# Gather ids loaded one tile ahead, and row transposes moved amid the second layer of the tile in front

## The reference, cut to what matters

```python
logits = x @ w_gate + modality_bias[modality_id]
e_idx = np.argmax(logits, axis=1)          # one expert per token
gate_w = probs[np.arange(N), e_idx]
for e in range(E):
    mask = e_idx == e
    h = np.maximum(x[mask] @ w1[e], 0.0)   # 512 -> 1024
    out[mask] = gate_w[mask, None] * (h @ w2[e])   # 1024 -> 512
```

## Time and profile before

| | |
|---|---|
| device time, 3 runs | 541.74, 542.89, 543.88 us (median 542.89) |
| profiled execution, its own time | 546.48 us |
| span of its trace | 544.8 us |
| PE busy | 519.8 us, 95% of the span |
| DVE, ACT, POOL busy | 215.7, 205.0, 220.1 us |
| mean granted clock of PE | 0.984 |

### The profile page before, as it was taken

How to read it: one execution, slowest core, us unless ns; L and a number is a source line. 1 busy time by engine, 2 the same in 40 slices (tenths; PEclk the granted TensorE clock), 3 DMA queues, 4 the chain that set the end, 5 groups by cost and what they waited for, 6 DMA issues and landing times. The chain is left out here.

```text
span 544.8 us, 9123 instructions
## 1 busy us (share of the span) xinstructions
PE 519.8 (95%) x2966; PEld 427.9 (79%) x2967; DVE 215.7 (40%) x418; ACT 205.0 (38%) x353; POOL 220.1 (40%) x222
## 2 busy tenths in 40 slices
PE   3999999999999999999999999999989999999993
PEld 2878888888788888878888888778768888888872
DVE  3433333333436322223623666362212472222892
ACT  0143333333343444444344655222212452222880
POOL 3675555454333365533347552130120161112461
PEclk9699999999999999999999999999989999999998
DMA  6944433430020700008100003105871111111110
GB/s 204 410 179 155 156 134 137 154 83 5 1 78 1 278 30 1 0 11 320 55 0 2 0 1 109 28 25 196 285 247 40 39 31 48 39 39 39 39 37 2
DMA packets 23017, 49.54 MB, mean 91 GB/s; under 512 B 8775, under 2 KB 10447, under 8 KB 22992
## 3 DMA queue, kind: packets, MB, share of 16 engines
q1 hardware_dynamic: 16496, 41.83, 21.7%
q0 software_dynamic: 2896, 7.36, 4.3%
q10 hardware_dynamic: 3600, 0.03, 0.3%
HBM read 42.80 MB, written 7.20 MB: 92 GB/s over the span
## 5 line engine op out<-in xcount | busy, mean ns | idle before, releaser
L520 POOL TENSOR_TENSOR wi_lo<-wd_raw,wi_hi 128x512 fp32r<-128x512 f32 x48 | 62.0, 1292 | 144.1 <-ACT wi_hi L660 144.0
L1245 PE MATMUL psum<-xT,wi_lo 128*128 128x512 f32 x192 | 77.3, 402 | 0.0
L1253 PE MATMUL psum<-wo_hi,act_lo 128*128 128x512 f32 x192 | 75.7, 394 | 0.4 <-DVE act_lo L911 0.4
L1247 PE MATMUL psum<-xT,wi_hi 128*128 128x512 f32 x192 | 75.0, 391 | 0.0
L1246 PE MATMUL psum<-xT,wi_hi 128*128 128x512 f32 x192 | 74.8, 390 | 0.0
L1255 PE MATMUL psum<-wo_hi,act_hi 128*128 128x512 f32 x192 | 74.8, 390 | 0.0
L1254 PE MATMUL psum<-wo_lo,act_hi 128*128 128x512 f32 x192 | 74.7, 389 | 0.0
L908 DVE SCALAR_TENSOR_TENSOR act_f<-psum,act_f 128x512 f32<-128x512 f32 x48 | 33.1, 690 | 95.4 <-ACT act_f L678 94.9
L678 ACT ACTIVATE act_f<-psum 128x512 f32<-128x512 f32 x48 | 28.6, 597 | 97.3 <-PE psum L1247 97.3
L525 POOL TENSOR_TENSOR wo_lo<-wd_raw,wo_hi 128x512 fp32r<-128x512 f32 x48 | 61.9, 1289 | 2.7 <-ACT wo_hi L665 2.7
L1334 PE MATMUL psum<-we_hi,he_lo 128*128 128x512 f32 x120 | 48.9, 408 | 4.2 <-issue 3.7
(11 more groups left out here) (167 smaller groups left out, 825.3 us busy)
## 6 DMA issues: line engine op xcount, KB each, us to landing
we_raw<-w_exp SPq DMA_DIRECT2D x32, 512.0 KB, 5.3
wd_raw<-w_dense SPq DMA_DIRECT2D x16, 512.0 KB, 5.4
qk_in<-attn_qk SPq DMA_DIRECT2D x10, 512.0 KB, 3.3
kv_in<-attn_kv SPq DMA_DIRECT2D x10, 512.0 KB, 4.2
x_d<-x_sb SPq DMA_DIRECT2D x12, 256.0 KB, 2.2
qk_more<-attn_qk SPq DMA_DIRECT2D x2, 512.0 KB, 6.4
kv_more<-attn_kv SPq DMA_DIRECT2D x2, 512.0 KB, 7.0
decay_mask<-pow_d SPq DMA_DIRECT2D x2, 256.0 KB, 3.7
```

What stands on the lines that cost most here:

```text
L520: nc.gpsimd.tensor_tensor(wi_lo[:, r, :], dense_raw(f, 0), wi_hi[:, r, :].bitcast(F32), ALU.subtract).then_inc(s_wil, 1)
L1245: nc.tensor.matmul(h, w_lo, hi, start=(c == 0), stop=False)
L1247: mm = nc.tensor.matmul(h, w_hi, hi, start=False, stop=(c == DC - 1))
L1253: nc.tensor.matmul(bank(ACC + i), lo, wo_hi[:, r, :], start=first, stop=False)
```

## The change

Ids. A second ids buffer, ids_n, receives the load from slots_d. POOL copies it to ids_g (a copy of 128x2) once the ids have landed and the gather before has landed, and gathers from ids_g. A new semaphore, s_idc, counts these copies. ACT's load of the ids of tile t+3 now waits for the copy for tile t+2 (before: the load for t+2 waited for the landing of gather t+1), and stands behind rows(t+1) on ACT. The table has one more entry (NTAB is 24, was 23), and one more load is made.

Transposes. In body, down(t, 0) is cut in two halves of 6 matmuls and transposes(t+1) stands between them; transposes(t+2) at the end is gone. So rows on ACT and rows_lo on DVE move from the end of iteration t (for tile t+2) into iteration t (for tile t+1): in a switch iteration they stand behind the first four weight pieces, in another at the iteration's start. For tiles 1 and 2 the same is written out. No rows beyond the last tile are transposed any more.

```diff
-NTAB = MAX_TILES + PRE + 1
+NTAB = MAX_TILES + PRE + 2
...
             def gather(t):
+                pool.wait_ge(s_ids, 16 * t)
+                pool.sem_inc(s_pass, 1)
+                pool.wait_ge(s_gat, 16 * t)
+                pool.sem_inc(s_pass, 1)
+                nc.gpsimd.tensor_copy(ids_g[:], ids_n[:]).then_inc(s_idc, 1)
+                pool.wait_ge(s_idc, t + 1)
+                pool.sem_inc(s_pass, 1)
                 pool.wait_ge(s_et, t)
-                pool.sem_inc(s_pass, 1)
-                pool.wait_ge(s_ids, 16 * t)
                 pool.sem_inc(s_pass, 1)
                 pool.indirect_dma_start(out=xg[:], ...
...
 ACT, ahead of the loop:
-            load_ids(ids_g, PRE, s_ids)
+            load_ids(ids_n, PRE, s_ids)
...
             rows(3)
-            act.wait_ge(s_gat, 16 * (PRE + 1))
-            load_ids(ids_g, PRE + 1, s_ids)
+            act.wait_ge(s_idc, PRE + 1)
+            load_ids(ids_n, PRE + 1, s_ids)
             hid(2, 1)
             relu(3, 0)
             hid(3, 0)
             relu(3, 1)
-            rows(4)
+            act.wait_ge(s_idc, PRE + 2)
+            load_ids(ids_n, PRE + 2, s_ids)
             with act.Fori(PRE, last) as t:
...
                     for f in range(4):
                         split(k1, f, 0, raw)
-                    act.wait_ge(s_gat, 16 * t + 32)
+                    rows(t + 1)
+                    act.wait_ge(s_idc, t + 3)
                     act.sem_inc(s_pass, 1)
-                    load_ids(ids_g, t + 2, s_ids)
+                    load_ids(ids_n, t + 3, s_ids)
                     hid(t, 1)
...
                 with act.Else():
-                    act.wait_ge(s_gat, 16 * t + 32)
+                    rows(t + 1)
+                    act.wait_ge(s_idc, t + 3)
                     act.sem_inc(s_pass, 1)
-                    load_ids(ids_g, t + 2, s_ids)
+                    load_ids(ids_n, t + 3, s_ids)
                     hid(t, 1)
...
                 relu(t + 1, 1)
-                rows(t + 2)
...
 DVE, in the loop:
                     for f in range(4):
                         split(k1, f, raw_of(k1))
+                    rows_lo(t + 1)
                     hid(t, 1)
...
                 with dve.Else():
+                    rows_lo(t + 1)
                     hid(t, 1)
                     evacuate_late(t)
                     hid(t + 1, 0)
-                rows_lo(t + 2)
...
 PE:
             up(0, 0, 1, range(2, DC))
-            transposes(1)
             ranks(BLOCKS - 1)
 
             def body(t, k, k_next):
-                down(t, k, 0)
+                down(t, k, 0, range(2))
+                transposes(t + 1)
+                down(t, k, 0, range(2, 4))
                 turn_hidden(t, 1)
                 up(t + 1, k_next, 0)
                 down(t, k, 1)
                 turn_hidden(t + 1, 0)
                 up(t + 1, k_next, 1)
-                transposes(t + 2)
```

More of the change, by code:

```diff
@@ L201, in fused_program @@
         ids_pre = sb("ids_pre", [P, PRE, 2], I32)
+        ids_n = sb("ids_n", [P, 2], I32)
         ids_g = sb("ids_g", [P, 2], I32)
@@ L294, in fused_program @@
         s_ids = sem("gather_ids_loaded")
+        s_idc = sem("gather_ids_copied")
         s_gat = sem("rows_gathered")
@@ L625, in split @@
                                         ALU.subtract).then_inc(s_el2[0], 1)
+            pool.sem_inc(s_idc, PRE)
             scatter_early(0)
@@ L1154, in _ @@
             hid(3, 0)
-            rows_lo(4)
             last = dve.value_load(tab[0:1, LAST_:LAST_ + 1], min_val=PRE + MIN_TILES - 1, max_val=PRE + MAX_TILES - 1)
@@ L1437, in _ @@
             t = PRE - 1
-            down(t, 0, 0)
+            down(t, 0, 0, range(2))
+            transposes(t + 1)
+            down(t, 0, 0, range(2, 4))
             turn_hidden(t, 1)
```

## The result

| | before | changed |
|---|---|---|
| device time, median (runs) | 542.32 us (4: 541.44, 541.74, 542.89, 543.88) | 550.94 us (4: 548.98, 550.91, 550.98, 553.94) |
| ratio, 95% interval | 1 | 1.0145 [1.0109, 1.0182] |
| profiled execution | 546.48 us, span 544.8 | 553.94 us, span 552.2 |

The change makes the kernel 1.45% slower by the ratio, which is 7.9 us; the medians lie 8.6 us apart. +3.5 was forecast.

A forecast was written before the change was run, and what follows sets the result against it. PE was taken as the bound, busy 519.8 of 544.8 us. Terms 0.5 - 4.6 + 1.5 + 0 + 6.1 = +3.5 on the median 542.89 gave 546.4 us, own range 545.6 to 548, 8-in-10 range 542.5 to 551.

The forecast's parts named there:

- two rivals with chances of 0.10 and 0.09: Clock falls in the new waits, 548.0 to 552.7 (0.10); tile 4's stall not in timed runs, 549.5 to 551.0 (0.09).
- The switch iterations: Tiles 6, 12, 13: PE waits 1.9 us for xe_lo behind four weight pieces; with effects behind the switch, +6.1.
- The entry: Tiles 0 and 1: tile 1's transposes leave a wait and cost their time inside down, +0.5.
- Plain tiles at 12.33: Tiles without a switch: the new chain of 2.08 us fits under PE's cover of 2.17, so cost 0.
- The late gather: Tile 5's rows, needed later, at the middle of tile 4's down: two idle pieces and the slow clock go, -4.6.
- the stall at tile 4 is not in the timed runs: Rival: little to win, full price to pay, 549.5 to 551.0; a gather landing 1.0 earlier costs nothing. Chance 0.09.
- The wait for ids on ACT: Loop's first iteration: ACT waits for POOL's copy, hid(t, 1) queued behind it, +1.5, bounds 0 and 2.0.
- The counted wait: Tile 3's down, half 1: PE waits for he_lo because ACT's he_hi stands behind POOL's ids copy, +1.5.
- The clock: Rival: the clock falls in the new waits of 1.9, one to four falls, +1.6 to +6.3. Chance 0.10.
- the shorter end: Behind tile 13: no transposes any more, and a dummy tile's rows_lo ahead of the last he_lo goes, -0.2.

The follow-up runs named there:

- e11: The kernel before, unchanged, run and profiled a second time: 541.56 us, one execution.
- e1: Changed kernel with rows (ACT) and rows_lo (DVE) behind the first weight piece in switch iterations, not the fourth: 545.85 us, ratio 1.0060.
- e4: Changed kernel plus seven matmuls, result never read, in PE's wait ahead of tile 0's down: 551.03 us, ratio 1.0145.
- e12: The kernel before, unchanged, run and profiled a third time: 541.00 us, one execution.
- e6: Changed kernel with only its ids part kept; PE's order, rows and rows_lo as in the kernel before: 542.13 us, ratio 0.9980.
- e8: Changed kernel with the edits of e1, e4 and e7 together: 543.18 us, ratio 1.0007.
- e3: Changed kernel with tile 1's transposes back ahead of the rank matmuls, in the wait ahead of tile 0's down: 553.22 us, ratio 1.0174.
- e9: Changed kernel plus seven unread matmuls ahead of tile 0's down and seven ahead of the first layer in each switch iteration: 548.55 us, ratio 1.0123.
- e5: Changed kernel with only its transposes part kept; ids as in the kernel before (one buffer, no copy): 550.88 us, ratio 1.0150.
- e7: Changed kernel with ACT's load of the ids of tile t+3 moved to the end of iteration t: 551.36 us, ratio 1.0155.
- e2: Changed kernel with ACT's ids load and its wait for POOL's copy behind the hidden copy hid(t, 1): 553.70 us, ratio 1.0178.
- e10: e6 with the edit of e7, the ids load at the iteration's end: 542.24 us, ratio 1.0012.

## Why the prediction was right, and where it was off

Right in direction (slower, chance 0.67). The time, 550.94, is outside the forecast's own range (545.6 to 548) and only just inside the wide one, which ends at 551. That end was put there for two rivals with chances of 0.10 and 0.09, and a part of each came true; that the wide range held is luck and does not speak for the sum. By its steps:

*The switch iterations*, forecast at +2.2, +2.2 and +1.7. The waits stand where they were put, released by xe_lo. Without clock falls the iterations take 15.04, 15.02 and 14.64 against 12.73, 12.72 and 12.97 in e11: +2.3, +2.3 and +1.7, 6.3 in all against 6.1. e1 takes the waits away, and the falls behind them, and gives 5 us back. This step is shown.

*The entry*, forecast +0.5. Without the fall, tile 0 takes 13.36 (e4) against 12.78 in e11 and e12: +0.6, and +0.1 in tile 1. Right.

*Plain tiles at 12.33*, with 0.09 us of cover: 12.31 to 12.32, and 12.42 to 12.44 for those right behind a wait (tiles 1, 4 and 7). Right.

*The late gather*, forecast -4.6. It went, but it was mis-sized: I took the one profiled execution for the typical one. In e11 and e12 it is worth 2.0 to 2.3. The rival "the stall at tile 4 is not in the timed runs" was half true: a smaller stall is. Its condition was wrong as well: a gather that landed 1.0 earlier would have cost about 2 us and not nothing (an estimate from what follows). The 0.87 us that tile 4's rows cost ahead of tile 3's down in the first profile, which the prediction did not price, fit this. There the gather, issued at 381.77, landed 4.4 us later, 0.9 ahead of its transposes; with 2 us ahead (e6) there was no cost, with 0.23 late (e11) 2.05, with 1.1 late (tile 5's rows in the first profile) 3.00. A likely reason, argued and not shown, is that PE's sequencer waits for the gather and then still has the branch and the table loads of the loop before it, with nothing queued; the trace says only "issue" there. Where the same wait stands amid a down, in e8, rows that come 1.1 late cost 1.2 (13.51 for 12.32). In the changed kernel, where no transposes stand ahead of the loop's head, tile 2 to tile 3 took 12.32.

*The wait for ids on ACT*, forecast +1.5, at most 2.0. The mechanism is there, but it holds up more than the one wait that was counted: in the changed kernel 0.27 us ahead of the first layer, 2.76 ahead of tile 3's down, half 1, and 0.61 ahead of tile 4's down, where the scatter ids come late. Its size follows the landing of tile 5's ids. They took 5.7, 5.5, 5.1, 4.5 and 3.8 us in the changed kernel, e3, e4, e1 and e9, and tile 3's stretch, less 1.6 for the fall in e3 and e4, was 16.7, 16.0, 16.0, 15.1 and 14.4: 2.0 to 4.4 over 12.3. The counted wait alone was 1.56 in e1, where the ids took 4.5, so the working for it was right. How much of this is in the timed runs stays open: e5 and e7 have none of it, and are no faster. The Trainium skill ("DMA: Bandwidth & Descriptors", section "Anatomy of one DMA") gives its rule of about 2 us for a small transfer for the path by way of GpSimd, while ACT issues these loads; under this traffic most of them took longer.

*The clock*, not in the sum and given a chance of 0.10 as a rival. Here the sum put at nothing a term that was in every profile with the transposes moved, except e8 and e9. A fall costs 1.6 us (16.63 against 15.03 in a switch iteration, 14.92 against 13.36 at tile 0). Over the profiles of this study, ahead of tile 0: after 1.70 us of idle time the clock fell in 5 of 5 (changed kernel, e1, e2, e5, e7); after 1.28 in 0 of 6 (kernel before three times, e3, e6, e10). In e4, e8 and e9 unread matmuls fill that time, and it didn't fall either. Behind the waits of 1.85 to 1.89 in the switch iterations (changed kernel, e2, e3, e4, e5, e7) it fell in 2 of 6 at tile 6 and in 5 of 6 at tile 12; at tile 13, where the wait is 1.4 (1.86 in e7), in 0 of 6. That makes about 2.2 falls an execution, 3.5 us.

The timed runs say less. Each lists its mean granted clock: profiles without a fall have 0.995 to 0.997, those with two 0.988 and 0.989, those with three 0.986, so that a fall takes some 0.0033. The changed kernel's four runs have 0.989 to 0.992, mean 0.9902, and 57 later runs of the kernel before have a mean of 0.9947. That is about 1.4 falls more in an execution, or 2.2 us, an estimate from these means.

Sum of the measured terms: 0.7 for entry, 6.3 for switches, 2.2 for falls, less 2.1 for the gather and 0.2 for the shorter end: 6.9. The ids' term comes on top, nothing to 4.4; measured are 7.9 by the ratio (its interval is 5.9 to 9.9) and 8.6 by the medians. So the forecast of 3.5 fell short by two terms of like size, a gather's gain 2.5 us too large and a clock at nothing, while its largest term was right. How the falls and the ids' wait share the rest is not shown by a time, since e3, e4 and e9 do not separate from the changed kernel by their intervals. What is shown by times is that the loss is in the transposes part (e5 has all of it, e6 none), that the rows behind four weight pieces are the most of it (e1), and that the three mends together take nearly all of it away (e8).

## What to carry to other kernels

A step moved into a shared, in-order queue has to be looked at in every branch of the loop: here it fits by 0.09 us in plain tiles and stands behind four weight pieces in three iterations of eleven, and those three decide. Where PE waits, count the clock as well as the wait: in these traces waits of 1.3 to 1.6 us were followed by a fall once in 14 cases, and waits of 1.7 us and more in 15 of 23, at 1.6 us each, with great differences from place to place. And look at a second execution before a stall is put into a sum: the one first profiled may not be typical.

## What the runs showed of the hardware

- A load of 1 KB took 1.7 to 2.2 us in the kernel before and in the changed kernel once the first weights had come, with a DMA share of 0.3 or less. While weights flowed, at a share of 0.6 and more, it took anything from 2.1 (e9) to 6.0 us (e4).
- A wait for data just ahead of the loop's branch and its two table loads costs PE 1.8 to 2.1 us more than its own length: 2.05 us for rows 0.23 late (e11), 2.27 for 0.14 (e12), 3.00 for 1.1 (the first profile).
- POOL's copy of 128x2 takes 0.18 to 0.21 us, and the indirect DMA behind it starts 0.92 us after its end.
- Which wait is followed by a clock fall varies between executions of like kernels: at tile 6 two of six, at tile 12 five of six, with idle times equal within 0.04 us.
